# A fused attention and two-MLP kernel on one core: the opening stage reordered (sums of q and k, GpSimd's sums, per-head local scores, v's loads)

## What is computed

```python
q_d, k_d, v_d = (t.reshape(B, H, Sd, 4, D).mean(axis=3) for t in (q, k, v))
out_up = np.repeat(sm_attn(q_d, k_d, v_d), 4, axis=2)
mask = np.abs(pos[:, None] - pos[None, :]) < 4
out_local = softmax(where(mask, scale * q @ k.T, -1e9)) @ v
x = (out_up + out_local) laid out as (2304, 512)
y = ((x @ w_a) * (x @ w_b)) @ w_out
h = y @ w_in;  solu = h * softmax(h);  out = (layernorm(solu) * g_ln) @ w_out2
```

## Time and profile before

| | us |
|---|---|
| median of 3 runs | 837.2 |
| lowest and highest run | 833.18, 838.5 |
| profiled execution, its own time | 840.08 |
| its span | 838.3 |
| PE busy | 783.5 (93%) |
| DVE busy | 586.1 (70%) |
| ACT busy | 249.8 (30%) |
| POOL busy | 185.9 (22%) |

### The profile page before, as it was taken

The page is one execution under the profiler, slowest core; times in us unless marked ns, Lnnn a source line. Parts: engine busy times, 40 slices in busy tenths (PEclk is TensorE's granted clock), DMA queues, the critical chain, the costliest instruction groups (busy, mean ns, idle before and its releaser), DMA issues. The chain is left out here.

```text
span 838.3 us, 11870 instructions
## 1 busy us (share of the span) xinstructions
PE 783.5 (93%) x4392; PEld 715.3 (85%) x4392; DVE 586.1 (70%) x1012; ACT 249.8 (30%) x583; POOL 185.9 (22%) x143
## 2 busy tenths in 40 slices
PE   5769899799799979999989999999999999999997
PEld 5648889789799979989989999999887888888885
DVE  2579899979879896879688697212346766676663
ACT  4453434233133322133213222224412222222221
POOL 3455555308404230002000323121200000000000
PEclk9999999999899998999999999999999999999999
DMA  9999968465767674767555553356111011111110
GB/s 186 220 217 209 245 176 223 138 203 162 229 194 239 229 197 138 192 171 158 137 178 170 170 160 104 113 182 221 51 51 50 26 51 51 51 32 44 51 39 25
DMA packets 94682, 119.11 MB, mean 142 GB/s; under 512 B 17057, under 2 KB 56739, under 8 KB 94625
## 3 DMA queue, kind: packets, MB, share of 16 engines
q1 hardware_dynamic: 79904, 108.85, 46.4%
q10 hardware_dynamic: 14721, 9.51, 4.1%
HBM read 97.49 MB, written 20.84 MB: 141 GB/s over the span
## 5 line engine op out<-in xcount | busy, mean ns | idle before, releaser
L826 PE MATMUL psum<-x_hi,w_hi 128*128 128x384 f32 x576 | 201.5, 350 | 5.5 <-DVE x_lo L1321 5.4
L827 PE MATMUL psum<-x_lo,w_hi 128*128 128x384 f32 x576 | 195.7, 340 | 0.0
L828 PE MATMUL psum<-x_hi,w_lo 128*128 128x384 f32 x576 | 195.5, 339 | 0.0
L826 PEld LDWEIGHTS psum<-x_hi,w_hi 128*128 128x128 f32 x576 | 110.6, 192 | 10.5 <-issue 9.9
L827 PEld LDWEIGHTS psum<-x_lo,w_hi 128*128 128x128 f32 x576 | 110.6, 192 | 0.0
L828 PEld LDWEIGHTS psum<-x_hi,w_lo 128*128 128x128 f32 x576 | 110.4, 192 | 0.0
L1327 DVE TENSOR_TENSOR ab_f<-psum,a_sb 128x384 f32<-128x384 f32 x72 | 39.9, 554 | 99.8 <-PE psum L828 63.3
L826 PE MATMUL psum<-ab_hi,wo_hi 128*128 128x384 f32 x288 | 101.7, 353 | 3.6 <-issue 3.6
L828 PE MATMUL psum<-ab_hi,wo_lo 128*128 128x384 f32 x288 | 98.6, 343 | 0.0
L827 PE MATMUL psum<-ab_lo,wo_hi 128*128 128x384 f32 x288 | 98.5, 342 | 0.0
L1622 POOL TENSOR_TENSOR ab_lo<-ab_f,ab_hi 128x384 fp32r<-128x384 f32 x24 | 37.4, 1557 | 187.6 <-ACT ab_hi L1102 187.6
(11 more groups left out here) (139 smaller groups left out, 1300.2 us busy)
## 6 DMA issues: line engine op xcount, KB each, us to landing
wo_hi<-wo_hi_scratch SPq DMA_DIRECT2D x54, 256.0 KB, 2.7
wo_lo<-wo_lo_scratch SPq DMA_DIRECT2D x54, 256.0 KB, 3.1
k_u<-in_k SPq DMA_DIRECT2D x11, 576.0 KB
v_u<-in_v SPq DMA_DIRECT2D x11, 576.0 KB
k_u<-in_k SPq DMA_DIRECT2D x17, 288.0 KB
v_u<-in_v SPq DMA_DIRECT2D x17, 288.0 KB
raw<-in_v SPq DMA_DIRECT2D x8, 576.0 KB, 7.0
raw<-in_q SPq DMA_DIRECT2D x8, 576.0 KB, 9.2
```

The costliest lines, as they stand in the source:

```text
L826: mm(dst, wh, xh, start=first, stop=False, skip_group_check=not check)
L827: mm(dst, wh, xl, start=False, stop=False, skip_group_check=not check)
L828: last = mm(dst, wl, xh, start=False, stop=end, skip_group_check=not check)
```

## The change

- `qT` becomes one plain copy of the turned q (one ACT instruction on 128 partitions for two on 64), and the zero fill goes. `head_scores` makes twelve products with 64 rows each, one for each head, where it made six with 128 rows. The very first is made 128 columns wide.
- ACT issues no load of v before `head_qT(0)`: four of the seven follow it, three follow `head_qT(1)`. A one-element exponential stands ahead of all, so that the table is loaded there.
- DVE's four `head_pool` calls move up: (0, 0) ahead of `head_inverse(2)`, (0, 1) ahead of `head_inverse(3)`, (1, 0) ahead of `head_local(2)`. PE's `turn_qk` and ACT's `qk_copy` move up with them.
- POOL's sums for batch 1 get a wait each: those of v wait until the pooled scores of batch 0 are all scaled (`hp_normed` 4), those of q until the last low half of x is there (`x_lo_ready` 4).

```diff
-    qT = place("qT", [128, 2, LT, 128], FP32, o + 18432)
+    qT = place("qT", [128, 2, NT], FP32, o + 18432)
...
+                par = c % 2
                 for t in range(LT):
-
-                    last = mm(bank(2)[:, t * WIN:(t + 1) * WIN], qT[:, c % 2, t, :],
-                              kT[:, c % 2, t * QR:t * QR + WIN], start=True, stop=True)
+                    for h in range(2):
+                        rows = slice(h * D, (h + 1) * D)
+
+                        wide = 2 if t == 0 and h == 0 else 1
+                        last = mm(bank(2)[h * QR:(h + wide) * QR, t * WIN:(t + 1) * WIN],
+                                  qT[rows, par, t * QR:(t + wide) * QR], kT[rows, par, t * QR:t * QR + WIN],
+                                  start=True, stop=True)
...
             head_values(1)
+            turn_qk(0, 6)
             head_turn_p(2)
-            turn_qk(0, 6)
             turn_qk(1, 7)
             head_values(2)
+            turn_qk(2, 6)
             head_turn_p(3)
-            turn_qk(2, 6)
             turn_qk(3, 7)
...
-            def load_v_head():
-                for t in range(LT):
+            def load_v_head(first, last):
+                for t in range(first, last):
...
-                for h in range(2):
-                    rows = slice(h * D, (h + 1) * D)
-                    last = A(qT[rows, c % 2, :, h * QR:(h + 1) * QR],
-                             bank(0, NT)[rows].rearrange("p (t q) -> p t q", q=QR), ACT.Copy)
-                last.then_inc(s.qT_ready, 1)
+                A(qT[:, c % 2, :], bank(0, NT), ACT.Copy).then_inc(s.qT_ready, 1)
...
             act.wait_ge(s.pads_ready, 1)
-            load_v_head()
-            act.wait_ge(s.qT_cleared, 1)
+            A(loc_sum[:, 0, 0:1], exponent[:, :], ACT.Exp).then_inc(s.act_begun, 1)
             head_qT(0)
+            load_v_head(0, 3)
             head_qT(1)
+            load_v_head(3, LT)
             head_exp(0)
...
             head_pT(1)
+            qk_copy(0, 6)
             head_exp(3)
             head_pT(2)
-            qk_copy(0, 6)
             qk_copy(1, 7)
+            qk_copy(2, 6)
             head_pT(3)
-            qk_copy(2, 6)
             qk_copy(3, 7)
...
             head_kT(3)
+            head_pool(0, 0)
             head_inverse(2)
             head_mask(3)
             head_local(1)
+            head_pool(0, 1)
             head_inverse(3)
-            head_pool(0, 0)
-            head_pool(0, 1)
+            head_pool(1, 0)
             head_local(2)
-            head_pool(1, 0)
             head_pool(1, 1)
...
             for tau in (2, 0):
+
+                pool.wait_ge(s.hp_normed if tau == 2 else s.x_lo_ready, PPB)
                 for half in range(2):
                     pool_rows(1, tau, half)
```

More of the change, by code:

```diff
@@ L359, in build_program @@
         y_loaded1 out_stored0 out_stored1
-        ident_step ident_ready edge_ready band_ready pads_ready
-        h_turned qT_cleared qT_ready kT_ready h_scored h_masked h_exped h_inv_ready h_normed h_p_turned h_pT_ready h_x_mm
+        act_begun ident_step ident_ready edge_ready band_ready pads_ready
+        h_turned qT_ready kT_ready h_scored h_masked h_exped h_inv_ready h_normed h_p_turned h_pT_ready h_x_mm
         hp_scored hp_bias_ready hp_exped hp_normed hp_turned hp_pT_ready
@@ L986, in head_qT @@
                 at_least(act, s.h_scored, c - 1)
-                for h in range(2):
-                    rows = slice(h * D, (h + 1) * D)
-                    last = A(qT[rows, c % 2, :, h * QR:(h + 1) * QR],
-                             bank(0, NT)[rows].rearrange("p (t q) -> p t q", q=QR), ACT.Copy)
-                last.then_inc(s.qT_ready, 1)
+                A(qT[:, c % 2, :], bank(0, NT), ACT.Copy).then_inc(s.qT_ready, 1)
             def head_exp(c):
                 act.wait_ge(s.h_masked, c + 1)
+                if c == 0:
+                    act.wait_ge(s.act_begun, 1)
                 at_least(act, s.h_inv_ready, c - 1)
@@ L1560, in _ @@
             step = Chain(pool, s.ident_step)
+            G.memset(exponent[:, :], -0.5)
             G.memset(v_h[0:PAD + 1, 0, :], 0.0).then_inc(s.pads_ready, 1)
@@ L1563, in _ @@
             G.memset(kT[:, :, 0:PAD], 0.0)
-            G.memset(qT[:, :, :, :], 0.0).then_inc(s.qT_cleared, 1)
             G.affine_select(out=ident[:, :], in_=ident[:, :], compare_op=ALU.not_equal, fill=1.0,
@@ L1578, in _ @@
                             base=-PAD, pattern=[[1, WIN]], channel_multiplier=0).then_inc(s.band_ready, 1)
-            G.memset(exponent[:, :], -0.5)
             step.link(G.memset(edge[:, :, :, :], BIG))
```

## The result

| | before | changed |
|---|---|---|
| median, us | 837.8 | 848.2 |
| lowest to highest, us | 833.2 to 838.5 | 843.4 to 851.1 |
| span of the profiled execution, us | 838.3 | 849.3 |

The changed kernel takes 1.0122 times as long, with a 95% interval of 1.0076 to 1.0168. It is slower by about 10 us, where 6 us less was forecast.

The account below looks back on a forecast made before the run. PE busy 93%, with the head a relay in which no engine is full; 6.7 + 2.0 + 0.9 - 5.2 = 4.4, plus 1.6 back at 104 us, gives 6.0 off 837.2: 831.2 us, range 825.5 to 837.5.

Parts of the forecast that it names:

- The likeliest course: The prediction's own step-by-step forecast from the head to the end: 6.0 us gained, 831.2 us; chance 0.44, range 828.5 to 834.
- v's own landing: Head, values of pair 0: v needed at 18.2 us lands before that, and up to 2.4 us later is hidden.
- q's data lands late: Rival, head: q's raw rows land after 24.2 us and stall DVE, no gain if at 30.2; chance 0.06.
- pooled scores start: End of the head's relay: the pooled scores start at 38.0 us instead of 44.67, 6.7 us earlier.
- pooled scores to last pair scaled: Pooled part: without POOL's stalls of DVE the stretch of 8.76 us becomes 6.7, a gain of 2.0.
- to the last low half of x: Halves of x: q's sums go, v's sums come; the stretch of 11.0 us becomes about 10.1.
- to the first gate: Behind the last low half: q's sums stall DVE 5.6 us less 0.38 idle; first gate at 65.4, 4.4 earlier.
- The price of 3.3 us for this half of the change: POOL's moved sums: they cost DVE 9.4 us of stalls where they cost 6.1, losing 3.3.
- So here loads come 6.7 earlier: Weights of tile 0: w_out loads follow the head 6.7 us earlier, so gain after 104 us is 4.4 to 6.7.
- Scores without overlap: Rival, local scores: the two heads' products take 3.2 us instead of 1.8; gain 4.0, 833.2 us; chance 0.2.
- POOL's sums that cost less: Rival: POOL's moved sums fit DVE's pauses or the PE's lead covers them; gain 9.6 to 11, 827 us; chance 0.17.
- the case of slower: Whole kernel: slower by over 1%, which needs q's data at 38 us or later; chance 0.03.

Follow-up runs that it names:

- experiment 3: Changed kernel, but v's loads issued by SyncE in its own queue, behind k and ahead of the raw rows: 839.03 us, 1.0009.
- experiment 4: experiment 3 without POOL's two new waits ahead of the sums of batch 1: 839.3 us, 1.0009 against the kernel before.
- experiment 5: experiment 3 with SP's queue reordered, weights of later blocks ahead of the store of v's sums: 834.88 us, 0.9968 against the kernel before.
- experiment 9: experiment 5 with 32 of 96 partitions of batch 1's raw q and k rows loaded, 1.5 MB less: 828.51 us, 0.9907 against the kernel before.
- 1: Changed kernel with v's seven loads issued by ACT ahead of all its work again: 836.75 us, 0.9996 against the kernel before.
- 7: experiment 5 without POOL's two new waits: 835.3 us, 0.998 against the kernel before.
- number 11: experiment 3 with block-diagonal local scores again, six products of 128 rows per pair; one run for the head's marks, no time given.
- 10: Kernel before with SP's queue reordered and the same 1.5 MB of raw rows left out: 835.28 us, 0.9978.
- 6: Kernel before with only the reordering of SP's queue: 836.28 us, 0.9985.
- experiment 8: Changed kernel with SP holding back the raw rows until v has landed: 839.72 us, 1.0016 against the kernel before.

## Why the prediction was wrong

**The likeliest course, step by step.** Up to the values of pair 0 it held: q's copy at 4.45 (forecast 4.5), the first scores at 6.95 (6.4, with an upper bound of 7.75), `head_exp(0)` at 11.58 (11.6). The twelve products took 2.25 to 2.29 us; 1.8 was taken and 3.2 was the other bound, both estimates from rows of before, so it looks as if the two heads overlap in part. By the rule of the Trainium skill that the prediction cites ("TensorEngine Tiling (Array Packing)", section "Restrictions and Gotchas") they would have waited for each other; 2.25 doesn't bear this out in full. Then the step that failed:

*"v's own landing, before 18.2 at head_values(0), is hidden up to 2.4 us later."* The sentence gives v 2.4 us of cover and no price and no chance beyond it. By its issue alone v would have been in time. Before, the last load is issued at 6.5 and the queue of ACT moves its last pieces of v at 12.5 us; 5 us later is 17.5, ahead of 18.2. What the sentence took over without a reason is the length of the landing: 6 us behind the last issue before, 25 us in the changed kernel. The prediction had the right kind of thought for the wrong load: it asked what v's traffic does to the raw rows of q ("q's data lands late", 0.06), and didn't ask what the raw rows do to v. The rows of q took no harm; they were forecast at 24.2, landed at 23.7 in the changed kernel, and ended DVE's wait at 24.61 in experiment 3. v is the side that loses: at 256 B for 3 KB it has twelve times as many packets for its bytes. Rows of before that bear on it: from 8 to 12 us SP's queue moved 1640 packets and ACT's 1226, side by side, about one for one. There both held small packets, so this cost v little, and the number wasn't read.

**What stood behind that step was nearly right up to the first gate, once v was in time (experiment 3).** The relay came out step by step: DVE's sums of q and k ended at 31.3, 33.6 and 35.6 us, where 31.35, 33.75 and 35.8 were forecast, and the scores that took 2.3 us for 1.8 were mostly hidden behind the wait for q's rows. The stretches of the changed kernel and of experiment 3 against the forecast:

| us | before | forecast | changed | exp. 3 |
|---|---|---|---|---|
| pooled scores start | 44.67 | 38.0 | 54.73 | 37.83 |
| pooled scores to last pair scaled | 8.76 | 6.7 | 6.4 | 6.4 |
| to the last low half of x | 11.0 | 10.15 | 9.4 | 9.4 |
| to the first gate | 5.4 | 10.55 | 9.8 | 4.9 |
| first sum of tile 1 | 136.9 | 4.4 to 6.7 earlier | 149.5 | 137.1 |

POOL and DVE alternate as the forecast said. The timeline of the changed kernel, DVE and POOL:

```profile
56.06 0.17 DVE L1291 TENSOR_SCALAR hp_bias<-hp_max 96x2 f32<-96x2 f32 x1
...
70.65 2.21 POOL L1606 TENSOR_TENSOR raw<-raw 96x768 f32<-96x768 f32 x1 [3.18 <-DVE x_lo L1326]
71.09 3.74 DVE L1314 TENSOR_TENSOR w_lo<-w_raw,w_hi 128x512 fp32r<-128x512 f32 x2
```

The small operation in the pooled part takes 0.17 us, where before the four took 754 ns in the mean, and behind the last low half two `w_lo` take 3.74 us. The stretch to the first gate is 4.4 us longer than before; 5.2 was forecast. In experiment 3 the same stretch is not longer at all, 4.9 us, since there POOL's sums found no data when it was free:

```profile
57.47 2.00 POOL L1606 TENSOR_TENSOR raw<-raw 96x768 f32<-96x768 f32 x1 [6.91 <-DMA raw<-in_q]
```

It waits 6.91 us for the raw rows of q, though the wait that the change adds had been met. In experiment 4, which has no such wait, they wait 6.96 us for the same rows and start at 56.98, so 3 and 4 differ little. The price of 3.3 us for this half of the change was too high: from the pooled scores to the first gate the changed kernel takes 25.65 us, 25.14 before, where 27.4 was forecast, and experiments 3 and 4 take 20.8 and 20.5.

**The second step that failed:** *"So here loads come 6.7 earlier"*, at the weights of tile 0. The prediction took the store of v's sums in SP's queue as the cause of the wait in the earlier trace rows and let the loads follow the head. The view that speaks against it was in the page of before, in the slices of the span, 21 us each, where a digit is the busy share of the DMA engines in tenths:

```profile
DMA  9999968465767674767555553356111011111110
```

Five slices of 9, the first 105 us: the DMA engines have little room. Where they are full, loads can't come 6.7 us earlier if the bytes ahead of them don't. The windows view tells it in numbers, the kernel before and then experiment 3, each from 0 to 88.5 and on to 137 us, where the first sum of tile 1 stands in both:

```profile
0.00:88.50 88.50, 67.28 (x418) 56.96 (x418) 56.16 (x130) 36.65 (x112) 37.52 (x44) 1.00 0.97 208
88.50:137.00 48.50, 44.94 (x275) 41.72 (x275) 44.89 (x57) 21.69 (x49) 27.90 (x18) 0.93 0.82 204
```

```profile
0.00:88.50 88.50, 67.51 (x484) 56.30 (x484) 57.09 (x134) 33.94 (x109) 38.39 (x43) 0.97 0.94 211
88.50:137.00 48.50, 43.13 (x255) 39.12 (x256) 45.67 (x51) 21.17 (x48) 27.57 (x18) 0.87 0.83 198
```

The last two columns are the DMA share and GB/s. Up to 88.5 us the engines are 97% and 94% busy and move 88.5 x 208 = 18.4 MB and 88.5 x 211 = 18.7 MB; up to 137 us it is 18.4 + 48.5 x 204 = 28.3 MB and 18.7 + 48.5 x 198 = 28.3 MB. The same bytes by the same time, with a head that is 11.2 us shorter in one of them. That the bytes are the same at this mark says little by itself, since the program needs the same loads to get there; what says something is the share, near 1 up to 88.5 us. Behind it the share is 0.82 and 0.83, and the DMA engines are not full there. For the changed kernel the sum up to its own mark, 149.5 us:

```profile
0.00:100.00 100.00, 66.52 (x462) 55.02 (x463) 59.35 (x132) 35.31 (x112) 38.42 (x44) 0.97 0.87 184
100.00:149.50 49.50, 44.50 (x280) 40.70 (x278) 44.97 (x55) 20.20 (x47) 27.20 (x18) 0.97 0.80 202
```

That is 18.4 + 10.0 = 28.4 MB, again the same, at a share of 0.87 up to 100 us, where before it was 0.97 up to 88.5. What emptied the DMA engines is seen from 37 to 50 us, the changed kernel and then the kernel before:

```profile
37.00:50.00 13.00, 11.62 (x119) 9.75 (x120) 8.11 (x25) 7.14 (x31) 5.02 (x4) 1.00 0.19 53
```

```profile
37.00:50.00 13.00, 8.51 (x79) 6.57 (x78) 8.26 (x15) 5.01 (x15) 5.54 (x4) 1.00 0.80 186
```

A share of 0.19 for 0.80: the engines move 13 x (186 - 53) = 1.7 MB less, or 8 us at the 208 GB/s that the kernel before keeps up to 88.5 us. The reason is SP, which has nothing it may issue. SP's waits and POOL's timeline, the changed kernel:

```profile
SPq L457 <- POOL raw L1609: 19.7, 1, 19.7
```

```profile
42.32 0.89 POOL L1600 TENSOR_TENSOR p_loc<-p_loc,loc_inv 128x420 f32<-128x420 f32 x1 [21.06 <-DVE loc_inv L1252]
```

SP waits 19.7 us to store a sum of POOL; POOL stands 21.06 us at the scaling of the probabilities, behind the chain that stands for v. So the wait for v stops the stream of loads too. This explains why it comes through to the end in full, while a gain of the head does not: the stream can be held up by the head, and hardly hurried by it. How much of the lost gain is the bytes' and how much the order's isn't separated in full: experiment 5 gives 2.8 us at tile 1 by order alone, experiment 9 another 4.1 by bytes. The pooled scores are 10.1 us late, the first gate 10.6, tile 1 12.5, the end 11.0.

Without the first failed step the result would have been experiment 3's or 1's, 837 to 839, at the upper end of the range (837.5) or just above it and 6 to 8 us off the forecast; the first failed step made it 848.

**The rivals.** Scores without overlap: the time of the products lies between the two ends, and its share of the kernel's time stays open. POOL's sums that cost less: they did, in the changed kernel and by experiments 4 and 7, and at least in experiment 4 for a reason that the rival didn't name, the late rows of q. q's data late: didn't happen; but its mechanism, v's loads and the raw rows in each other's way, was the right one on the wrong side. It had 0.06, and the case of slower 0.03.

**What stays open.** The scores per head: number 11 is disturbed by the PE's pace. Of the 7.7 us that the first gate is earlier in experiment 9 than in 10 (61.13 for 68.79), 3.1 are left at tile 1, though ACT's waits for w_out are short in both (5.8 and 2.0 us): what takes the rest there wasn't found. Whether another order of the loads, with all bytes, would free more than the 1.4 us between experiments 5 and 6 wasn't tried.

## What to carry to other kernels

When a load is moved behind others, don't ask only how much later it is issued: look at the other queues that are full at that time, and compare packet sizes. A load of small packets that is soon needed must not run against a queue of large ones; put it ahead in the same queue, or hold the other back. And when a prologue is to be shortened, read the DMA share first: here it was near 1.0 up to 88.5 us, and a chain of compute that was 11.2 us shorter at 58.6 gave nothing that showed at 137. Expect such a gain to come through only in part, and look at the order of the loads and at their bytes before working on the chain.

## What the runs showed of the hardware that was not expected

Two DMA queues with work were served about one packet for one, with 3 KB against 256 B (302 and 256 in 4 us) and with 256 B on both sides (1640 and 1226 in 4 us, before). Three loads of 256 B pieces, 0.43 MB, issued from 10.1 to 11.5 us, landed at 36.8 against a queue of 3 KB rows; issued from 9.7 to 11.0 they landed by 15.8 us without it (experiment 8).

Products of two heads on different rows of the array, written to different partitions of one bank, took 2.25 us for twelve, where the earlier trace rows suggested 1.8 and no overlap would be 3.2. Both ends are estimates; that they overlap in part is read from them, and no run has the same products in two banks.

The same 24 records of values took 1.55 us in most runs and 0.92 in some, with the same code at that step. The windows view around them, experiment 3 (1.55) and experiment 8 (0.92):

```profile
18.00:28.00 10.00, 10.00 (x113) 8.81 (x113) 5.21 (x31) 3.26 (x16) 4.67 (x5) 1.00 1.03 250
```

```profile
18.00:21.00 3.00, 3.00 (x57) 2.79 (x54) 1.46 (x13) 0.31 (x1) 0.02 (x1) 1.00 1.02 279
```

The granted clock is 1.00 in both, the level of 2.4 GHz, so here it doesn't tell them apart. Later in experiment 8 it falls to 0.50, the level of 1.2 GHz, and there the 24 records take 1.55 us (timeline, then the windows view):

```profile
33.42 1.55 PE L700 MATMUL psum<-pT_loc,v_h 70*64 70x64 f32 x24
```

```profile
33.00:35.00 2.00, 1.97 (x27) 1.56 (x26) 1.96 (x3) 0.70 (x1) 1.50 (x1) 0.50 1.12 222
```

So 1.55 us is the pace at a granted 0.50 in experiment 8 and the pace at a granted 1.00 in the head of experiment 3. Why the rows of the head show 1.00 beside the slower pace was not found; until it is, a granted 1.00 in the head doesn't prove the faster one.
